# Bucket codes from six projections per head, with the high parts of q and k stacked by GpSimd in a score operand's rows

## Time and profile before

| what | value |
|---|---|
| time, median of 3 runs | 1008.08 us (1007.16 to 1009.15) |
| time of the profiled execution | 1007.33 us |
| its span, first to last instruction | 1005.5 us |
| granted TensorE clock, mean | 1.000 |
| DVE busy, ACT busy, POOL busy, of the span | 63%, 46%, 41% |
| ACT `pT_hi` copy (L711), mean of 96 | 803 ns |
| DVE `pT_lo` (L1005), mean of 96 | 946 ns |
| DMA `q_main<-q_cross`, 192 KB, issue to landing, median | 2.7 us |

### The profile page before, as it was taken

The page is one execution under the profiler, slowest core; times in us unless marked ns, Lnnn a source line. Parts: engine busy times, 40 slices in busy tenths (PEclk is TensorE's granted clock), DMA queues, the critical chain, the costliest instruction groups (busy, mean ns, idle before and its releaser), DMA issues.

```text
span 1005.5 us, 15929 instructions
## 1 busy us (share of the span) xinstructions
PE 994.0 (99%) x5526; PEld 922.2 (92%) x5526; DVE 637.1 (63%) x964; ACT 461.9 (46%) x853; POOL 411.9 (41%) x416
## 2 busy tenths in 40 slices
PE   9999999999999999999999999999999999999998
PEld 6879999999988999999998998989989899898997
DVE  6348999999996997398765354453634536345342
ACT  4248888888886544354452150421504224042230
POOL 4021434285457993494355160341604416043130
PEclk9999999999999999999999999999999999999999
DMA  6323333333332221011020110201101011010102
GB/s 242 95 72 95 96 112 107 94 102 94 98 87 79 63 70 36 22 43 43 1 64 22 42 43 1 63 22 43 43 3 61 21 42 42 13 50 21 42 16 110
DMA packets 58925, 60.58 MB, mean 60 GB/s; under 512 B 7808, under 2 KB 46848, under 8 KB 58880
## 3 DMA queue, kind: packets, MB, share of 16 engines
q1 hardware_dynamic: 58880, 60.00, 20.1%
HBM read 44.20 MB, written 3.19 MB: 47 GB/s over the span
## 4 chain that ended last, share of the span: by engine, by line
PE 90%; DVE 5%; ACT 2%; issue 2%; DMA 1%; POOL 0%; SPq 0%; DVEq 0%; ACTq 0%; POOLq 0%
PE ps L288 23%; PE ps L289 22%; PE ps L290 22%; PE ps L1390 6%; PE ps L1377 3%; PE ps L1403 3%; PE ps L1379 3%; PE ps L1405 3%; PE ps L1355 2%; PE ps L1350 2%; DVE w_lo L1020 1%; DVE hid_lo L1145 1%; DVE pT_lo L1005 1%; DMA w_raw<-in_moe_w 1%; PE ps L1309 1%
## 5 line engine op out<-in xcount | busy, mean ns | idle before, releaser
L615 POOL TENSOR_TENSOR v_sum<-kept,kept 128x384 f32<-128x384 f32 x48 | 52.3, 1089 | 292.0 <-ACT kept L800 292.0
L1277 DVE SCALAR_TENSOR_TENSOR acc<-ps,gate,acc 128x512 f32<-128x512 f32 x96 | 72.0, 750 | 134.8 <-PE ps L290 134.8
L800 ACT COPY kept<-ps 128x384 f32<-128x384 f32 x144 | 64.4, 481 | 200.8 <-PE ps L290 200.2
L290 PE MATMUL ps<-v_hi,hid_lo 128*128 128x512 f32 x384 | 149.6, 390 | 0.0
L289 PE MATMUL ps<-v_lo,hid_hi 128*128 128x512 f32 x384 | 149.5, 389 | 0.0
L288 PE MATMUL ps<-v_hi,hid_hi 128*128 128x512 f32 x384 | 149.4, 389 | 0.0
L987 DVE TENSOR_SCALAR_CACHE_REDUCE expo<-ps 128x768 f32<-128x768 f32 x96 | 91.6, 954 | 15.2 <-PE ps L1379 14.9
L1264 DVE SCALAR_TENSOR_TENSOR hid_lo<-c,hid_hi 128x384 fp32r<-128x384 f32 x96 | 64.5, 685 | 46.2 <-ACT hid_hi L921 19.1
L703 ACT ACTIVATE expo<-expo,neg_max 128x768 f32<-128x768 f32 x96 | 90.6, 944 | 6.5 <-DVE expo L987 5.0
L711 ACT CAST pT_hi<-ps 128x768 fp32r<-128x768 f32 x96 | 76.9, 803 | 32.0 <-PE ps L1390 31.6
L1005 DVE TENSOR_TENSOR pT_lo<-ps,pT_hi 128x768 fp32r<-128x768 f32 x96 | 90.4, 946 | 1.5 <-ACT pT_hi L711 1.5
(11 more groups left out here) (160 smaller groups left out, 2513.9 us busy)
## 6 DMA issues: line engine op xcount, KB each, us to landing
w_raw<-in_moe_w SPq DMA_DIRECT2D x64, 128.0 KB, 2.4
e_raw<-in_moe_w SPq DMA_DIRECT2D x64, 128.0 KB, 2.4
v_raw<-in_moe_w SPq DMA_DIRECT2D x32, 256.0 KB, 3.4
w_raw<-in_moe_w SPq DMA_DIRECT2D x8, 512.0 KB, 3.7
raw_q<-in_q SPq DMA_DIRECT2D x16, 192.0 KB, 2.9
raw_k<-in_k SPq DMA_DIRECT2D x16, 192.0 KB, 2.9
raw_v<-in_v SPq DMA_DIRECT2D x16, 192.0 KB, 2.7
q_main<-q_cross SPq DMA_DIRECT2D x16, 192.0 KB, 2.7
```

The costliest lines, as they stand in the source:

```text
L290: return nc.tensor.matmul(out_ps, lhs_lo, rhs_hi, start=False, stop=stop, skip_group_check=onto)
L615: nc.gpsimd.tensor_tensor(v_sum[:, :], kept[s][1][:, :], kept[s][2][:, :], ALU.add).then_inc(v_done, 1)
L800: nc.scalar.copy(kept[s][n][:, :], ps[4 * s + n][:, 0:HALF]).then_inc(kept_done, 1)
L1277: nc.vector.scalar_tensor_tensor(acc[:, t, :], ps[4 * ((h + t // 4) % 2) + t % 4], gate_f[:, bass.ds(t * E + e, 1)], acc[:, t, :], ALU.mul ...
```

## The change

The projection by the low part of `proj` needs only the high parts of q and k. The kernel after stacks q high (rows 0 to 63, from `q_cross`) and k high (rows 64 to 127, from `k_cross`) in `q_main`, by two copies of 64 x 768 on POOL. One matmul for each half of the tokens then does the low-part projection of both. Step 4 is six matmuls: four (`project_parts`), and later two. The k high rows in `q_main` are overwritten by the one-hot rows afterwards, as before. The DMA of q high to `q_main` is gone. On PE the last two matmuls stand after the transposes of tile 5 and the scores of tile (1, 2); on DVE the bits come after the scaling of tile (1, 2). POOL's order in a head becomes: split q, split k, split v, the two stacking copies, both `x_scale`, `first_parts`.

```diff
 # SP
 def move_high(m, s):
     sp.wait_ge(prep_copied, 4 * m + 4)
-    move(s, (q_main[s][0:DH, :], q_cross[s][0:DH, :]), (k_main[s][0:DH, :], k_cross[s][DH:P, :]))
+    move(s, (k_main[s][0:DH, :], k_cross[s][DH:P, :]))
 # POOL
+def stack_highs(m, s, values):
+    pool.wait_ge(v_split, values)
+    for part, (rows, src) in enumerate(((slice(0, DH), q_cross), (slice(DH, P), k_cross))):
+        pool.wait_ge(prep_copied, 4 * m + 2 * part + 2)
+        held()
+        nc.gpsimd.tensor_copy(q_main[s][rows, :], src[s][rows, :].bitcast(F32)).then_inc(highs_stacked, 1)
+        pool.wait_ge(highs_stacked, 2 * m + part + 1)
+    held()
...
 split_v(0, 0, 0, True)
+for s in range(2):
+    stack_highs(s, s, 1)
...
-for t in range(TILES):
-    if t == 0 and not last:
-        split_q(m + 2, i + 1, s, False)
-    if t == 1 and not last:
-        split_k(m + 2, s)
-    if t in (2, 4) and s == 0 and not first:
-        x_scale(i - 1, t // 2 - 1)
-    if t == 3 and s == 0:
-        split_v(m + 1, i, 1, first)
-    if t == 3 and s == 1 and not last:
-        split_v(m + 1, i + 1, 0, False)
+if not last:
+    split_q(m + 2, i + 1, s, False)
+    split_k(m + 2, s)
+if s == 0:
+    split_v(m + 1, i, 1, first)
+elif not last:
+    split_v(m + 1, i + 1, 0, False)
+if not last:
+    stack_highs(m + 2, s, m + 2)
+if s == 0 and not first:
+    x_scale(i - 1, 0)
+    x_scale(i - 1, 1)
 for step in parts[s:s + 1]:
...
 # DVE
     pT_low(6 * m + 4, 4)
+    scale(1, 2)
     encode(2, 4)
-    scale(1, 2)
     pT_low(6 * m + 5, 5)
 # PE
 elif j == 4:
-    for n, w in enumerate(proj_w):
-        half = slice((n // 4) * HALF, (n // 4 + 1) * HALF)
-        last = nc.tensor.matmul(ps_prep[:, 0:HALF], w[:, :],
-                                (q_cross if n % 4 < 2 else k_cross)[s][:, half],
-                                start=n == 0, stop=n == 7)
+    pe.wait_ge(highs_stacked, 2 * m + 2)
+    for h in range(2):
+        last = nc.tensor.matmul(ps_prep[:, 0:HALF], proj_w[3 * h + 2][:, :],
+                                q_main[s][:, h * HALF:(h + 1) * HALF], start=False, stop=h == 1)
+def project_parts(m, s):
+    pe.wait_ge(prep_copied, 4 * m + 4)
+    for h in range(2):
+        for n, src in enumerate((q_cross, k_cross)):
+            nc.tensor.matmul(ps_prep[:, 0:HALF], proj_w[3 * h + n][:, :],
+                             src[s][:, h * HALF:(h + 1) * HALF], start=h + n == 0, stop=False)
...
     values(0, 0, 0, 1)
-    prepare(2, 4)
+    project(2)
     transpose(5)
     score(1, 2)
+    prepare(2, 4)
     values(0, 0, 1, 5)
     prepare(2, 5)
```

More of the change, by code:

```diff
@@ L178, in build_program @@
         k_parts = [place(f"k_parts{s}", [P, TILES, P], F32R, prep_at) for s in range(2)]
-        proj_w = [place(f"proj_w{n}", [P, P], F32R, prep_at) for n in range(8)]
+        proj_w = [place(f"proj_w{n}", [P, P], F32R, prep_at) for n in range(6)]
         onehot = place("onehot", [P, S], F32R, prep_at)
@@ L247, in build_program @@
         prep_mm, prep_copied, prep_coded = sem("prep_mm"), sem("prep_copied"), sem("prep_coded")
+        prep_open, highs_stacked = sem("prep_open"), sem("highs_stacked")
         score_mm, score_scaled, exp_done = sem("score_mm"), sem("score_scaled"), sem("exp_done")
@@ L420, in _ @@
             move_onehots(HEADS - 1, 1)
-            sp.wait_ge(stacks_moved[1], 64 * PAIRS)
+            sp.wait_ge(stacks_moved[1], 48 * PAIRS)
             sp.wait_ge(prep_mm, GROUPS * HEADS)
@@ L505, in _ @@
             nc.gpsimd.memset(ident[:, :], 0.0).then_inc(zeros_set, 1)
-            for n in range(8):
+            for n in range(6):
                 nc.gpsimd.memset(proj_w[n][:, :].bitcast(F32), 0.0).then_inc(zeros_set, 1)
@@ L1062, in constants @@
                 dve.wait_ge(const_loaded, 16 * (4 + B))
-                dve.wait_ge(zeros_set, 9)
+                dve.wait_ge(zeros_set, 7)
                 nc.vector.tensor_copy(code[:, :, :], code_f[:, :, :]).then_inc(code_ready, 1)
@@ L1066, in constants @@
                 for n in range(4):
-                    nc.vector.tensor_copy(proj_w[2 * n][:, cols[n]], proj_f[:, :]).then_inc(proj_hi_ready, 1)
+                    nc.vector.tensor_copy(proj_w[n + n // 2][:, cols[n]], proj_f[:, :]).then_inc(proj_hi_ready, 1)
                 dve.wait_ge(proj_hi_ready, 4)
                 for n in range(4):
-                    nc.vector.tensor_tensor(proj_w[2 * n + 1][:, cols[n]], proj_f[:, :],
-                                            proj_w[2 * n][:, cols[n]].bitcast(F32), ALU.subtract)\
+                    rows = slice(0, DH) if n % 2 == 0 else slice(DH, P)
+                    nc.vector.tensor_tensor(proj_w[3 * (n // 2) + 2][rows, cols[n]], proj_f[rows, :],
+                                            proj_w[n + n // 2][rows, cols[n]].bitcast(F32), ALU.subtract)\
                         .then_inc(proj_ready, 1)
@@ L1084, in first_code @@
                 if n == GROUPS + 5:
-                    dve.wait_ge(stacks_moved[0], 64)
+                    dve.wait_ge(stacks_moved[0], 48)
                 if n % GROUPS >= 4:
@@ L1338, in prep @@
                     pe.wait_ge(prep_coded, 3 * m)
-                elif 1 <= j <= 4:
+                elif 1 <= j < 4:
                     pe.wait_ge(prep_copied, 4 * m + j)
@@ L1366, in first_prep @@
                     pe.wait_ge(code_ready, 1)
+                if n % GROUPS == 4:
+                    project_parts(n // GROUPS, n // GROUPS)
                 prep(n // GROUPS, n // GROUPS, n % GROUPS, n < GROUPS)
@@ L1371, in scores @@
                 if t == 0:
-                    pe.wait_ge(stacks_moved[s], 64 * (i + 1))
+                    pe.wait_ge(stacks_moved[s], 48 * (i + 1))
                 if not first:
@@ L1427, in prepare, with project @@
                             prep(m + ahead, at(ahead)[1], j, False)
+                    def project(ahead):
+                        if not (last and s + ahead > 1):
+                            project_parts(m + ahead, at(ahead)[1])
                     def transpose(t):
```

## The result

The changed kernel takes 1004.94 us (median of 7 executions, 1002.23 to 1006.44), the one before 1008.51 in the same comparison (median of 7, 1007.16 to 1010.01). The ratio is 0.996, with a 95% interval of 0.9949 to 0.9971, so it is faster by 0.4%, about 4 us. The forecast was 1003.3. The profiled execution of after took 1005.19 us with a span of 1003.4; that of before had 1005.5, so these two traces show a difference of 2.1 us, and it is they that are compared here.

The account below looks back on a forecast made before the run. PE, busy for 994.0 of 1005.5 us, was taken as the bound. The terms 5.6 + 2.3 - 2.9 - 0.4 - 0.15 gave 4.45 us less, 1002.9 or 1003.6 by starting time; the forecast was 1003.3, range 1000.6 to 1007.4.

Parts of the forecast that it names:

- Matmuls removed: PE's projections in 16 heads: two fewer of 0.175 us each, 5.6 us less in all, a head 15.06 us.
- Three collisions: DVE's guards in heads 9, 11 and 13 no longer meet POOL's `first_parts`: 2.3 us less.
- the margin of 0.09 us between copy and guard: POOL's first stacking copy in a head would be done 0.09 us before DVE's guard starts, so they never meet.
- PE's wait for q: POOL's longer queue in head 8 delays the split of q; PE waits 2.9 us, bounds 2.4 and 3.9.
- DVE's margins: DVE's scaling of tile (1, 1) and its bits would just be ready for PE, by 0.05 and 0.08 us.
- The charge of 0.4 us: Loss allowed for DVE's narrow margins: 0.03 us in each of 14 heads, 0.4 us in all.
- The first rival: The saving turns into PE's waits on DVE: 1005.4 us if half is lost, 1007.8 if all; 25%.
- The second rival: The guard collides with the first stacking copy in every head: 0.9 us in each of 14, 1016 us; 9%.
- Head 1, 0.15 us: In head 1's preparation PE reaches the moved matmuls before the k stacking copy is done and loses 0.15 us.

Follow-up runs that it names:

- e5_double: Kernel after with the two stacked matmuls issued twice, so eight projections a head again; 1009.63 us, ratio 1.0012 to the kernel before.
- e2_before_noguard: Kernel before without the guard's addition on DVE, the reciprocal reading the sums directly; 1005.96 us, ratio 0.9973 to the kernel before.
- e1_spread: Kernel after with the four POOL operations of step 0 of `first_parts` dealt over heads 8 and 9; 1000.47 us, ratio 0.9919 to the kernel before.
- e6: Kernel after with the first stacking copy replaced by a two-input addition of q high to itself; 1010.32 us, ratio 1.0023 to the kernel before.
- e8_olddve: Kernel after with DVE's old order, the bits ahead of the scaling of tile (1, 2); 1005.37 us, ratio 0.9968 to the kernel before.
- e4: Kernel after with step 0 of `first_parts` dealt over two heads and without the guard addition; 1001.07 us, ratio 0.9923 to the kernel before.
- e7: Kernel after with one of the four POOL operations of step 0 moved from head 8 to head 9; 1000.35 us, ratio 0.9923 to the kernel before.

## Why the prediction was right, and where it was not

- **Matmuls removed, 5.6 us: shown.** 15.41 became 15.07 a head, and e5_double gives the same 0.35 back.
- **Three collisions, 2.3 us: shown.** All guards of after but head 15's are 0.15 to 0.24 us long, and in the kernel before it is the guard that cost this (e2_before_noguard: 1.49 us for two of the three on the chain). The reason given for it, copies of 0.82 us and `first_parts` behind them, is in the rows. But the margin of 0.09 us between copy and guard isn't there: the copy starts 0.19 us behind the split, since it waits for its result, where I had taken 0.06, and the guard begins before its end, by 0.10 us in head 9 (218.31 and 218.41) and by 0.22 in head 1. Guards do meet the copy, at its very end, and lose up to 0.07 us, which PE doesn't feel. This part came out right by less than the precision with which it was worked out.
- **PE's wait for q, 2.9 us: shown,** 2.87, from seven durations read in the rows of before. e1_spread takes it away.
- **Its second half was missing.** The step said that nothing behind the wait could use the time; it did not ask what the wait does to the clock. In the traced execution the stretch behind it ran at a granted clock of 0.53, and with the 0.17 to start again this cost 1.8 us more. Five of the seven executions of after have a mean clock of 0.998 and not 1.0, which is what one such stretch would give; they take 1003.78 to 1006.44, the other two 1002.99 and 1002.23, and the forecast of 1003.3 lies between the groups. That this is most of the 1.6 us between forecast and median is likely but not shown: only one of the seven was traced, and the mean clock is a weak sign. Five of the 44 executions of before in the experiments have 0.998 too, and in e6 the two executions at 1.0 take 1010.26 and 1010.77, as much as the others.
- **Head 15's guard, 0.9 us, was not seen.** I followed guards up to head 13 since `first_parts` ends there, but the POOL work of the weights goes on behind it, and it had a 0.58 us guard in before already. It was visible.
- **DVE's margins.** The charge of 0.4 us was too much: heads take 15.06 to 15.07. The first rival did not come. But the reason that I gave, that moving the bits keeps the margin, has fallen with e8_olddve: the old order costs 0.05 to 0.08 us in every second head. I had counted DVE's waits ahead of the point as fixed and had not seen that those behind it (0.2 to 0.3 us each) give way. The reason given for this rival also has a misread row: the guard of 0.67 us lies in the window in which DVE is busy for 13.88 us, not in that with 14.28.
- **The second rival** had the right mechanism: an operation on 64 x 768 with one tensor read twice takes 1.46 us and costs 0.4 to 0.5 us a head. Its own price, 0.9 us a head, was for 1.86 us, a length that no run reached. It was to decide from a copy of 1.3 us; at 1.46 the whole is 1010.32, slower than before, which bears that out.
- **Head 1, 0.15 us:** the only wait for a stacking copy in the attention, 0.3 us of a weight load, is there; it delays the matmul by 0.15 us. As forecast.

From trace to trace the sum said 4.45 us less and 2.1 came: 1.8 and 0.9 that were missed, less the 0.4 charged for nothing, are that difference of 2.3. From median to median 3.6 us came (1008.51 to 1004.94), nearer to the forecast than the traces are. The traced execution of before lies 1.2 us under its median and that of after 0.25 above, so part of this closeness is luck.

**Open.** Why PE waits on `kept` in the gates for 2.7 or 3.2 us in all, the longest 1.1, in the profiled executions of e1 to e4 and e6, for 1.5 or 1.6 in those of e5 and e7, and for only 0.8 or 1.1 in those of e8, after and before, is not settled. What I suppose: DVE's, POOL's and ACT's operations there have little slack, and a shift of 1 us in the attention changes which comes first. No run tried it. It limits what can be said of any change of 1 us in this kernel.

## What to carry to other kernels

When work is put ahead of other work on an in-order engine, add up the queue behind it up to the next thing that the bounding engine needs; if TensorE stands still for it, look at the granted clock behind the wait too: here a wait of 2.87 us cost 1.6 us more where the clock fell. Spread the burst (here one or two of four 1.8 us operations moved one head on) before anything else is tuned. And look for tiny VectorE operations whose duration varies from 0.15 to 1.8 us: they mark collisions with GpSimd. What one costs is what it is held for less the margin behind it: guards of 0.67 us cost nothing in before, those of 1.81 us 0.75 to 0.78, and in e6 those of 0.68 to 0.87 cost 0.4 to 0.5, since after has less margin.

## What the runs showed of the hardware that was not expected

- **The clock after a stop.** Behind 2.87 us without work TensorE's granted clock was 0.53 over 3.6 us of full work, then 1.00. Behind 2.90, 2.54 and 1.88 us it fell too; behind 2.66, 1.67 and 0.99 us it didn't, so a stop shorter than another can be the one that costs. The Trainium skill (TensorE: Matmul & The Clock Gate, "What's actually happening") says that the clock has these two levels alone and follows how busy TensorE has been; the windows agree, with the lower level showing only when TensorE had begun again.
- **A cast on GpSimd takes as long for 64 partitions as for 128.** A cast of 64 x 768 takes 0.82 us, that of 128 x 768 took 0.82. With two inputs it is 1.84 for 128 x 768 of different data and 1.46 for 64 x 768 of one tensor read twice; which of the two differences makes the 0.4 us was not tried.
- **A GpSimd operation that waits for the one before** starts mostly 0.17 to 0.26 us later, and 0.30 us or more where the next is an `x_scale`.
- **A cast on POOL holds the guard too,** not only an operation with two inputs: in heads 1, 3 and 7 of after the guard takes 0.24, 0.20 and 0.20 us instead of 0.17 and ends 0.02 or 0.03 us behind the first stacking copy.
